# Encoder kernel on one core: small first inverse, TensorE kept at work before the projection, PSUM ring counted on at the end, tile 2's scores behind unit 0

## Chip, cores and metric

One Trainium2 chip, one core of it. The metric is the device time of one execution in microseconds (us). The kernel before takes 1320.02 us, the median of three runs.

## The reference

Pooled attention, then two feed-forward layers, all in float32. With q of 12288 rows by 128, kv of 384 x 32 positions by 128:

```
kv_pool = kv.reshape(B, 96, 4, 8, 4, C).mean(axis=(2, 4))     # 768 keys
k = v = kv_pool.reshape(B, 768, C) @ w_sr
a = softmax((q @ k.T) / sqrt(C))                              # sum + 1e-9
x = a @ v                                                     # 12288 x 128
h = x @ w_in1                                                 # 12288 x 2048
g = where(h >= 1, h, where(h <= -1, 0, (h + 1) ** 2 / 4))
y = g @ w_out1                                                # 12288 x 128
h2 = y @ w_in2
out = (h2 * sigmoid(1.702 * h2)) @ w_out2
```

## The kernel before

All tensors lie transposed: 128 channels or keys on the partitions, query rows along the free dimension. A query tile is T = 512 rows, there are NT = 24. Keys come in KC = 6 chunks of 128. The 2048 hidden features are taken as U = 8 units of 256, two blocks of 128 side by side in a 128x1024 PSUM buffer. A unit has a running number n = 8 * tile + unit.

A product that must be accurate is three TensorE passes of 512 columns (`three_passes`, L449 to L451): both operands are split in an upper part (float32r) and a lower remainder, and upper*upper, upper*lower and lower*upper are added up. The uppers are copies on ScalarE or VectorE; the lowers are subtractions, most of them on GpSimd (`lower`, L367: q_lo, k_lo, w_lo, g_lo, pt_lo). Early products (projections, values of tiles 0 to 2, layer 1's output for tile 0) are plain float32 instead, two instructions each.

**Order of the work.** There is no planner; each engine runs a program written out by hand, with semaphores between them. Iteration `it` holds, on TensorE, a block with the scores of tile `it` and the values of tile `it - 2`, and then eight steps k. A step has up to four parts: `layer_in` of layer 2 (h2), `layer_in` of layer 1 (h1, unit n = 8*it + k - 18), `layer_out` of layer 1 (two units behind) and `layer_out` of layer 2. ScalarE does Relu and Square of h1, and two passes of Gelu of h2; VectorE makes g1_hi and g1 (`unit_upper` L970, `unit_full` L979); GpSimd g1_lo and g2_lo. The last 11 units' g2_lo are VectorE's (TAIL). After the ramp, iterations 6 to 21 are a loop, and 22 to 27 are written out.

**PSUM.** Three buffers of 128x1024 form `ps_ring`; two of 128x512 (ps_y1, ps_y2) accumulate the layer outputs. h2 and h1 of step k take ring buffers `(2 + 2*k) % 3` and `(3 + 2*k) % 3`. The scores of a block use buffer 0, its values buffer 1. Since 16 is not a multiple of 3, the turn starts anew with each iteration: h1 of k = 7 and h2 of the next k = 0 both use buffer 2, with the block between them. In iterations 26 and 27 there is no block.

**Softmax.** Scores are copied to SBUF; VectorE takes the maximum over the keys in three `maximum` reductions and `fold_maximum`, which ends in max_turned; SP's queue writes it to DRAM and reads it back spread over all partitions (`spread_max`, key_max); VectorE's three `shift`s subtract it, ScalarE takes the exponentials, `add_keys` and `invert` make the inverse of the sums, which goes the same way through DRAM (`spread_inv`). `normalise` multiplies the values by it (x_sb), and x_hi and x_lo follow. Tile 0 goes another way: its maximum is spread by TensorE (`subtract_maximum` L503, with masked rows of `ident`), and its sums too, by one product with a matrix of ones, after which VectorE inverts all 128x512 of them (`normalise_first`).

**The ramp on each engine.** TensorE: key projection of the first 512 keys, value projection, scores of tile 0 (chunks 0 to 3), projections of the last 256 keys, chunks 4 and 5, scores of tile 1, `subtract_maximum`, values of tile 0 with the spread sums between chunks 3 and 4, steps of "iteration 2" (units 0 to 5), values of tile 1, scores of tiles 2 and 3, steps of iteration 3, and iteration 4. Layer 1's output of tile 1 (unit 8) can't start before y_lo of tile 0 has been taken out of ps_y1. VectorE sums the kv windows in 12 groups of 64 keys as they arrive, and then follows the order in the code at the end of its block. GpSimd: q_lo, k_lo, q_lo, w_lo of w_in1, then from x_lo of tile 0 on the other weights. ScalarE makes w_hi of w_in1 between the last value projection and the copies of tile 1's scores (`evacuate`).

## Time and profile before

| | |
|---|---|
| Median of three runs | 1320.02 us (1318.38 to 1321.22) |
| Profiled execution: time | 1320.54 us |
| Profiled execution: span | 1318.7 us |
| Mean granted TensorE clock | 0.994 |
| TensorE busy | 1274.6 us, 97% |
| GpSimd busy | 1145.5 us, 87% |
| ScalarE busy | 1007.7 us, 76% |
| VectorE busy | 1002.1 us, 76% |

PE is TensorE's matmuls, PEld its weight loads (which overlap them), DVE is VectorE, ACT ScalarE, POOL GpSimd, SPq the queue of SyncE. Times of the trace are us from the span's start. In a row of a time line, the first number is the start, the second how long the instruction or a run of like ones took, `xN` their count, and a bracket tells how long the engine was idle before, and which instruction ended the wait. Drawn matmul durations overlap; the distance between two starts is what a pass costs. A row of the table of stretches gives for each of PE, PEld, DVE, ACT and POOL the busy time and the instructions in brackets, then the granted TensorE clock, the DMA engines' share and GB/s.

### The profile page before, as it was taken

To read this page: it belongs to the slowest core of one execution; us is meant where nothing else is said; L and a number is where in the kernel's file an instruction comes from. 1 tells how busy PE (TensorE), PEld (TensorE's weight loads), DVE (VectorE), ACT (ScalarE), POOL (GpSimd) and SP (SyncE) were. 2 spreads that over 40 slices of the span, in tenths; PEclk is the share of its full clock that TensorE was granted. 3 is DMA by queue.
4 is the path that set the end of the run, shared out by engine and by line. 5 is a ranking of instruction groups with operands and counts; after the bars stand their busy time and mean duration, and the time that the engine had idled before them with its cause. 6 is when DMAs were issued, how large, how long until landed. Compare 5 with 4: busy or idle time off the path is not lost.

```text
span 1318.7 us, 16960 instructions
## 1 busy us (share of the span) xinstructions
PE 1274.6 (97%) x5468; PEld 1028.7 (78%) x5468; DVE 1002.1 (76%) x1146; ACT 1007.7 (76%) x1070; POOL 1145.5 (87%) x477
## 2 busy tenths in 40 slices
PE   4888999999999999999999999999999999999988
PEld 3446888888888888888888888888888888878866
DVE  6878779779788787797787887877978878756433
ACT  2567788887878887878778788878788787886756
POOL 2337999999999999999999999999999999998760
PEclk9998999999999999999999999999999999999999
DMA  9000000000010010000000000100000000000000
GB/s 347 22 17 24 17 17 32 16 17 17 16 32 16 16 32 16 16 31 17 16 16 16 32 16 16 32 16 16 28 20 16 16 17 25 9 17 17 1 8 17
DMA packets 18258, 35.72 MB, mean 27 GB/s; under 512 B 3248, under 2 KB 3376, under 8 KB 17968
## 3 DMA queue, kind: packets, MB, share of 16 engines
q1 hardware_dynamic: 18224, 35.30, 8.2%
q8 instruction: 18, 0.29, 0.1%
q14 instruction: 16, 0.13, 0.0%
HBM read 28.90 MB, written 6.39 MB: 27 GB/s over the span
## 4 chain that ended last, share of the span: by engine, by line
PE 82%; POOL 7%; issue 6%; DVE 3%; ACT 1%; DMA 1%; SPq 0%; POOLq 0%; ACTq 0%; DVEq 0%
PE ps_ring L449 16%; PE ps_ring L450 15%; PE ps_ring L451 15%; PE ps_y L449 11%; PE ps_y L451 11%; PE ps_y L450 11%; POOL g_lo L367 5%; POOL pt_lo L367 2%; DMA kv_sb<-in_kv_t 1%; PE ps_y L527 1%; PE ps_y L552 1%; DVE g L979 0%; DVE s_third L926 0%; DVE part_max L865 0%; DVE g_hi L970 0%
## 5 line engine op out<-in xcount | busy, mean ns | idle before, releaser
L367 POOL TENSOR_TENSOR g_lo<-g,g_hi 128x1024 fp32r<-128x1024 f32 x365 | 930.1, 2578 | 92.1 <-DVE g L979 86.7
L970 DVE SCALAR_TENSOR_TENSOR g_hi<-g,ps_ring 128x1024 fp32r<-128x1024 f32 x184 | 224.1, 1218 | 151.6 <-ACT g L768 150.7
L749 ACT ACTIVATE g<-ps_ring 128x1024 f32<-128x1024 f32 x192 | 197.2, 1027 | 182.8 <-PE ps_ring L451 178.6
L449 PE MATMUL ps_y<-g_hi,w_hi 128*128 128x512 f32 x752 | 297.0, 395 | 11.8 <-DVE y_lo L824 7.0
L450 PE MATMUL ps_y<-g_lo,w_hi 128*128 128x512 f32 x752 | 293.7, 391 | 0.0
L451 PE MATMUL ps_y<-g_hi,w_lo 128*128 128x512 f32 x752 | 293.7, 391 | 0.0
L979 DVE SCALAR_TENSOR_TENSOR g<-g,ps_ring 128x1024 f32<-128x1024 f32 x192 | 233.0, 1213 | 9.6 <-ACT g L768 9.6
L761 ACT ACTIVATE g<-ps_ring 128x1024 f32<-128x1024 f32 x192 | 197.9, 1031 | 17.0 <-PE ps_ring L451 10.4
L768 ACT ACTIVATE g<-g 128x1024 f32<-128x1024 f32 x192 | 204.2, 1063 | 5.4
L751 ACT ACTIVATE g_hi<-ps_ring 128x1024 fp32r<-128x1024 f32 x192 | 195.9, 1020 | 5.1 <-PE ps_y L451 5.1
L449 PEld LDWEIGHTS ps_y<-g_hi,w_hi 128*128 128x128 f32 x752 | 141.4, 188 | 49.7 <-POOL g_lo L367 10.6
L451 PEld LDWEIGHTS ps_y<-g_hi,w_lo 128*128 128x128 f32 x752 | 141.7, 188 | 29.9
L450 PEld LDWEIGHTS ps_y<-g_lo,w_hi 128*128 128x128 f32 x752 | 141.7, 188 | 28.3
L367 POOL TENSOR_TENSOR pt_lo<-s_sb,pt_hi 128x1024 fp32r<-128x1024 f32 x63 | 159.1, 2559 | 0.0
L449 PE MATMUL ps_ring<-x_hi,w_hi 128*128 128x512 f32 x384 | 153.5, 400 | 5.2 <-DVE x_lo L824 4.5
L449 PE MATMUL ps_ring<-y_hi,w_hi 128*128 128x512 f32 x384 | 150.9, 393 | 4.8 <-DVE g L979 4.8
L450 PE MATMUL ps_ring<-y_lo,w_hi 128*128 128x512 f32 x384 | 150.6, 392 | 0.0
L451 PE MATMUL ps_ring<-y_hi,w_lo 128*128 128x512 f32 x384 | 150.3, 391 | 0.0
L450 PE MATMUL ps_ring<-x_lo,w_hi 128*128 128x512 f32 x384 | 150.1, 391 | 0.0
L451 PE MATMUL ps_ring<-x_hi,w_lo 128*128 128x512 f32 x384 | 150.0, 391 | 0.0
L926 DVE TENSOR_TENSOR s_sb<-s_sb,key_max 128x1024 f32<-128x1024 f32 x66 | 124.5, 1889 | 0.0
L848 DVE COPY s_sb<-ps_ring 128x512 f32<-128x512 f32 x120 | 81.0, 689 | 54.6 <-PE ps_ring L451 54.6
(114 smaller groups left out, 1675.4 us busy)
## 6 DMA issues: line engine op xcount, KB each, us to landing
kv_sb<-in_kv_t SPq DMA_DIRECT2D x12, 512.0 KB, 8.6
q_sb<-in_q_t SPq DMA_DIRECT2D x24, 256.0 KB, 3.6
out_t<-y_sb SPq DMA_DIRECT2D x24, 256.0 KB, 3.6
key_max<-max_row SPq DMA_DIRECT2D x23, 256.0 KB, 3.4
inv_sum<-inv_row SPq DMA_DIRECT2D x23, 256.0 KB, 3.3
w_raw<-in_moe_w_in SPq DMA_DIRECT2D x2, 1024.0 KB, 17.7
max_row<-max_turned SPq DMA_DIRECT2D x23, 2.0 KB, 1.3
inv_row<-inv_turned SPq DMA_DIRECT2D x23, 2.0 KB, 1.3
```

The lines of the kernel that those rows point to most:

```text
L367: return nc.gpsimd.tensor_tensor(dst, src, upper.bitcast(F32), ALU.subtract)
L449: nc.tensor.matmul(dst, l_hi, r_hi, start=start, stop=False)
L450: nc.tensor.matmul(dst, l_hi, r_lo, start=False, stop=False)
L451: return nc.tensor.matmul(dst, l_lo, r_hi, start=False, stop=stop)
L749: nc.scalar.activation(g2[:, slot, :], ps_h2(k), ACT.Gelu_apprx_sigmoid).then_inc(g2_done, 1)
L751: nc.scalar.activation(g2_hi[:, slot, :], ps_h2(k), ACT.Gelu_apprx_sigmoid).then_inc(g2_hi_done, 1)
L761: nc.scalar.activation(g, ps_h1(k), ACT.Relu, bias=0.5, scale=0.5).then_inc(relu_done, 1)
L768: nc.scalar.activation(g, g, ACT.Square).then_inc(square_done, 1)
L848: nc.vector.tensor_copy(s_sb[:, half, c, :], ps_s(it, c)).then_inc(s_evac, 1)
L926: nc.vector.tensor_tensor(pair, pair, key_max[:, :].unsqueeze(1).to_broadcast([P, 2, T]), ALU.subtract).then_inc(shifted, 1)
L970: nc.vector.scalar_tensor_tensor(out=g1_hi[:, uu % 2, :], in0=g1[:, uu % 2, :], scalar=1.0, in1=ps_h1(k), op0=ALU.min, op1=ALU.max).then_i ...
L979: nc.vector.scalar_tensor_tensor(out=g, in0=g, scalar=1.0, in1=ps_h1(k), op0=ALU.min, op1=ALU.max).then_inc(g1_done, 1)
```

## The change

1. TensorE: ahead of the first key projection, behind each of window groups 4 to 7, two products of w_k with the first 256 window sums into an unused buffer. The result is not read.
2. Projection and scores of tile 0: k_lo of the first 512 keys in two halves; the projection of the last keys comes ahead of chunk 3; VectorE takes the maximum of chunk 0 alone, before k_lo of the last keys. w_hi of w_in1 is made by GpSimd, its first half before the maximum and its second after the maximum is masked. `ident` is 128x128.
3. First inverse: the key sums are added over the partitions by four products with one column each (128x4), inverted there, multiplied into the identity, and spread by one product with ones; ScalarE copies the result to inv_sum.
4. Unit 0 (`first_unit`) starts on x_hi, and adds the part with x_lo at the end. It needs only half of w_lo of w_in1.
5. Tile 2's scores stand behind unit 0, ahead of units 1 to 5, no longer behind tile 1's values. The maximum, shifts, key sums and exponentials of tile 2, and the order on SP, move forward to match.
6. Iterations 26 and 27 (`blockless`) count the ring on from iteration 25; h2 there waits for the unit before, not for the newest.
7. pt_lo of the last tile is made by VectorE (`last_probs_lower`), not GpSimd.

```diff
@@ names @@
+        def ring_turn(it, k):
+            return k + U * (it - NT - 1) if blockless(it) else k
+        def ps_h2(it, k):
+            return ps_ring[:, (2 + 2 * ring_turn(it, k)) % 3, :]
+        def ps_h1(it, k):
+            return ps_ring[:, (3 + 2 * ring_turn(it, k)) % 3, :]
+        def blockless(it):
+            return isinstance(it, int) and it >= NT + 2
@@ sync @@
+            spread_max(2)
             spread_inv(1)
-            spread_max(2)
@@ gpsimd @@
             def iteration(it, half):
-                if is_tile(it - 1):
+                if is_tile(it - 1) and not is_number(it, NT):
                     for p in range(PAIRS):
                         probs_lower(it - 1, 1 - half, p)
...
-            lower(k_lo[:, 0:FIRST_KEYS], k_sb[:, :], k_hi[:, 0:FIRST_KEYS]).then_inc(k_lo_first, 1)
+            for b in range(2):
+                keys = slice(b * FIRST_KEYS // 2, (b + 1) * FIRST_KEYS // 2)
+                lower(k_lo[:, keys], k_sb[:, keys], k_hi[:, keys]).then_inc(k_lo_first, 1)
             q_lower(1, q1_lo[:, :], q_sb[:, 1, :], q1_hi[:, :])
+            w_upper(0, 0)
             w_lower(0, 0)
+            pool.wait_ge(max_masked, 2)
+            w_upper(0, 1)
             w_lower(0, 1)
+            q_lower(2, q2_lo[:, :], q2_sb[:, :], q2_hi[:, :])
             pool.wait_ge(x_lo_done, 1)
@@ tensor @@
-                nc.tensor.matmul(ps_y2[:, :], ones[:, :], key_sums[:, 4, :], start=True,
+                for j in range(QUADS):
+                    last = nc.tensor.matmul(ps_y2[:, j:j + 1], key_sums[:, 4, j * P:(j + 1) * P], ones[:, 0:1],
+                                            start=True, stop=True)
+                last.then_inc(first_summed, 1)
+            def spread_inverse():
+                pe.wait_ge(inverse_masked, 1)
+                nc.tensor.matmul(ps_y2[:, :], ones[:, :], key_sums[:, 0, :], start=True,
                                  stop=True).then_inc(sums_spread, 1)
+            def first_unit(dst):
+                pe.wait_ge(w_lo_done[0], 1)
+                pe.wait_ge(x_hi_done, 1)
+                for d in range(2):
+                    f = slice(d * P, (d + 1) * P)
+                    half = dst[:, d * T:(d + 1) * T]
+                    nc.tensor.matmul(half, w_hi[:, f], x_hi[:, 0, :], start=True, stop=False)
+                    nc.tensor.matmul(half, w_lo[:, f], x_hi[:, 0, :], start=False, stop=False)
+                pe.wait_ge(x_lo_done, 1)
+                for d in range(2):
+                    f = slice(d * P, (d + 1) * P)
+                    last = nc.tensor.matmul(dst[:, d * T:(d + 1) * T], w_hi[:, f], x_lo[:, 0, :], start=False, stop=True)
+                last.then_inc(h1_ready, 1)
...
-                    if k == 0:
-                        at_least(pe, g1_done, it * U - 18 if unit(it, k - 1, FIRST1)[0] else NT * U)
+                    if blockless(it):
+                        pe.wait_ge(g1_done, min(it * U + k - 19, NT * U))
+                    elif k == 0:
+                        at_least(pe, g1_done, it * U - 18)
...
-                        at_least(pe, g1_done, it * U + k - 19 if layer1 else NT * U)
+                        at_least(pe, g1_done, it * U + k - 19)
...
             pe.wait_ge(w_scaled, 2)
+            for g in range(4, FIRST_GROUPS):
+                pe.wait_ge(summed, g)
+                for _ in range(2):
+                    nc.tensor.matmul(ps_k[:, 3, 0:4 * GK], w_k[:, :], window_sum[:, 0:4 * GK], start=True, stop=True)
             project_k(0)
             project_v(0)
-            for c in range(FIRST_CHUNKS):
+            for c in range(FIRST_CHUNKS - 1):
                 score_chunk(0, c)
             project_k(1)
+            score_chunk(0, FIRST_CHUNKS - 1)
             project_v(1)
...
-            spread_sums()
-            for c in range(4, KC):
-                value_chunk(0, c)
-            for k in range(U):
+            sum_first_keys()
+            value_chunk(0, 4)
+            spread_inverse()
+            value_chunk(0, 5)
+            for k in range(3):
                 step(2, 0, k)
-            values_then_scores(1, 2, 3)
+            for c in range(KC):
+                score_chunk(2, c)
+            pe.wait_ge(s_early, 2 * KC)
+            for k in range(3, U):
+                step(2, 0, k)
+            values_then_scores(1, 3)
@@ scalar @@
-            w_upper(0)
             evacuate(1, 1)
             for p in range(PAIRS):
                 exponential_first(p)
+            act.wait_ge(sums_spread, 1)
+            copy(inv_sum[:, :], ps_y2[:, :]).then_inc(inverse_copied, 1)
             copy(v_hi[:, :, :], v_sb[:, :, :]).then_inc(v_hi_done, 1)
             act.wait_ge(q2_loaded, 16)
             copy(q2_hi[:, :], q2_sb[:, :]).then_inc(q_hi_done, 1)
             step(2, 0, 2)
+            evacuate(2, 0)
@@ vector @@
+            def invert_first():
+                dve.wait_ge(first_summed, 1)
+                nc.vector.tensor_scalar(inv_first[:, :], ps_y2[:, 0:QUADS], 1e-9, None, ALU.add).then_inc(first_eps, 1)
+                dve.wait_ge(first_eps, 1)
+                nc.vector.reciprocal(inv_first[:, :], inv_first[:, :]).then_inc(first_inverse, 1)
...
-                nc.vector.tensor_scalar(inv_sum[:, :], ps_y2[:, :], 1e-9, None, ALU.add).then_inc(eps_added, 1)
-                nc.vector.reciprocal(inv_sum[:, :], inv_sum[:, :]).then_inc(inverted, 1)
...
+                if is_number(it, NT):
+                    for p in range(PAIRS):
+                        last_probs_lower(it - 1, 1 - half, p)
...
             unit_full(2, 2)
+            for p in range(PAIRS):
+                maximum(2, 0, p)
             unit_full(2, 3)
             shift(1, 1, 0)
             unit_full(2, 4)
             shift(1, 1, 1)
             shift(1, 1, 2)
             unit_full(2, 5)
+            fold_maximum(2)
...
             unit_full(2, 7)
-            for p in range(PAIRS):
-                maximum(2, 0, p)
-            fold_maximum(2)
             normalise(1)
             x_lower(1, 1)
+            for p in range(PAIRS):
+                shift(2, 0, p)
```

In iteration 3, VectorE's `shift`s of tile 2 fall away at k = 1 and 2, `fold_maximum(3)` moves from k = 2 to 1, the key sums of tile 2 from k = 4 to 2 and 3 (y_lo of tile 0 comes at the start of k = 3), and `invert(2)` from k = 5 to 4; ScalarE's three exponentials of tile 2 stand behind steps 0, 1 and 2 in place of all behind step 3.

## Rows read from the trace of the kernel before

**Rows 1.** The page, shares of the engines (busy us, share of the span, instructions)
```profile
PE 1274.6 (97%) x5468; PEld 1028.7 (78%) x5468; DVE 1002.1 (76%) x1146; ACT 1007.7 (76%) x1070; POOL 1145.5 (87%) x477
```

**Rows 2.** Table of stretches, 200 to 400 us
```profile
200.00:400.00 200.00, 200.00 (x881) 164.55 (x880) 161.02 (x187) 161.17 (x170) 192.29 (x79) 1.00 0.07 22
```

**Rows 3.** Time line of TensorE, ramp: start, us, instruction, idle before and its releaser
```profile
16.32 2.05 PE L456 MATMUL ps_k<-window_sum,w_k 128*128 128x512 f32 x2 [16.32 <-DVE window_sum L834]
...
20.97 0.77 PE L449 MATMUL ps_ring<-q_hi,k_hi 128*128 128x512 f32 x1 [0.90 <-POOL k_lo L367]
...
25.72 0.59 PE L456 MATMUL ps_k<-window_sum,w_k 128*128 128x256 f32 x2
26.15 0.61 PE L462 MATMUL ps_v<-w_v,window_sum 128*128 128x128 f32 x4
27.25 0.50 PE L449 MATMUL ps_ring<-q_hi,k_hi 128*128 128x512 f32 x1 [0.49 <-DVE k_lo L824]
...
33.93 1.62 PE L503 MATMUL ps_ring<-spread_hi,minus_ones 128*128 128x512 f32 x6 [0.33 <-DVE spread_hi L890]
...
48.22 0.50 PE L449 MATMUL ps_ring<-x_hi,w_hi 128*128 128x512 f32 x1 [4.50 <-DVE x_lo L824]
...
80.84 0.50 PE L449 MATMUL ps_ring<-x_hi,w_hi 128*128 128x512 f32 x1 [0.69 <-ACT s_sb L680]
...
101.95 0.80 PE L449 MATMUL ps_y<-g_hi,w_hi 128*128 128x512 f32 x1 [7.04 <-DVE y_lo L824]
...
115.10 0.47 PE L449 MATMUL ps_y<-g_hi,w_hi 128*128 128x512 f32 x1 [0.97 <-POOL g_lo L367]
```

**Rows 4.** Time line of ScalarE: score copies of tile 2
```profile
71.19 1.30 ACT L680 ACTIVATE s_third<-ps_ring 128x512 f32<-128x512 f32 x2 [3.67 <-PE ps_ring L451]
```

**Rows 5.** Time line of VectorE in the ramp
```profile
8.56 12.73 DVE L834 TENSOR_REDUCE window_sum<-kv_sb 128x64 f32<-128x1024 f32 x10 [0.89 <-DMA kv_sb<-in_kv_t]
...
31.52 1.47 DVE L885 CAST row_hi<-row_max 32x16 fp32r<-32x16 f32 x1
...
42.76 3.35 DVE L915 RECIPROCAL inv_sum<-inv_sum 128x512 f32<-128x512 f32 x1
...
62.80 3.49 DVE L932 TRANSPOSE_TENSOR_REDUCE part_sum<-s_sb 128x32 f32<-128x1024 f32 x3
...
69.78 0.24 DVE L950 RECIPROCAL row_sum<-row_sum 32x16 f32<-32x16 f32 x1
70.05 0.20 DVE L953 STREAM_TRANSPOSE inv_turned<-row_sum 32x32 f32<-32x32 f32 x1
...
90.99 1.21 DVE L926 TENSOR_TENSOR s_third<-s_third,key_max 128x1024 f32<-128x1024 f32 x1
...
95.51 4.50 DVE L926 TENSOR_TENSOR s_third<-s_third,key_max 128x1024 f32<-128x1024 f32 x2
```

**Rows 6.** Time line of GpSimd in the ramp
```profile
19.56 1.26 POOL L367 TENSOR_TENSOR k_lo<-k_sb,k_hi 128x512 fp32r<-128x512 f32 x1 [10.48 <-ACT k_sb L680]
...
104.23 2.38 POOL L367 TENSOR_TENSOR g_lo<-g,g_hi 128x1024 fp32r<-128x1024 f32 x1 [5.30 <-DVE g L979]
```

**Rows 7.** The page, DMA issues: count, KB each, us to landing
```profile
inv_sum<-inv_row SPq DMA_DIRECT2D x23, 256.0 KB, 3.3
...
inv_row<-inv_turned SPq DMA_DIRECT2D x23, 2.0 KB, 1.3
```

**Rows 8.** Time line of TensorE in the tail
```profile
1178.65 0.68 PE L449 MATMUL ps_y<-g_hi,w_hi 128*128 128x512 f32 x1 [2.02 <-POOL g_lo L367]
...
1264.51 0.80 PE L449 MATMUL ps_ring<-y_hi,w_hi 128*128 128x512 f32 x1 [2.35 <-DVE g L979]
...
1279.53 0.47 PE L449 MATMUL ps_ring<-y_hi,w_hi 128*128 128x512 f32 x1 [2.44 <-DVE g L979]
```

**Rows 9.** Time line of GpSimd in the tail
```profile
1168.69 7.59 POOL L367 TENSOR_TENSOR pt_lo<-s_sb,pt_hi 128x1024 fp32r<-128x1024 f32 x3
```

**Rows 10.** Time line of VectorE in the tail
```profile
1283.17 1.23 DVE L824 TENSOR_TENSOR g_lo<-g,g_hi 128x1024 fp32r<-128x1024 f32 x1 [3.78 <-ACT g_hi L751]
```

More of the change, by code:

```diff
@@ L963, in x_lower, with last_probs_lower @@
                 lower(x_lo[:, half, :], x_sb[:, :], x_hi[:, half, :]).then_inc(x_lo_done, 1)
+            def last_probs_lower(t, slot, p):
+                chunks = slice(2 * p, 2 * p + 2)
+                dve.wait_ge(pt_hi_done, (t - WHOLE) * PAIRS + (p + 1))
+                dve.wait_ge(pv_done, (t - 1) * KC + (2 * p + 2))
+                lower(pt_lo[:, chunks, :], s_sb[:, slot, chunks, :], pt_hi[:, chunks, :]).then_inc(pt_lo_last, 1)
             def unit_upper(it, k):
@@ L1054, in _ @@
             unit_full(2, 7)
-            for p in range(PAIRS):
-                maximum(2, 0, p)
-            fold_maximum(2)
             normalise(1)
             x_lower(1, 1)
+            for p in range(PAIRS):
+                shift(2, 0, p)
             for k in range(U):
```

130 lines of the change are left out of this document (73 added, 57 removed).

## The prediction

> **What bounds the kernel now.** I read the page first for the shares of the engines, then the table of stretches, then the time line of each engine through the first 145 us and the last 160 us. TensorE is busy for 97% of the span [rows 1]. In the table of stretches it is busy for all of 200 to 400 us, 881 instructions in 200 us, so one full 512-column pass in 0.227 us, at a granted clock of 1.00; GpSimd has 192.3 us of the 200 and follows close behind [rows 2]. The middle of the kernel is therefore TensorE's own work. The change leaves the loop's instructions as they are, so whatever it does to the time is made where TensorE stands or runs at the lower of its levels (1.2 instead of 2.4 GHz): the ramp to 115 us, and the tail from 1165 us. The time line of TensorE names these places. In the ramp: scores of tile 0 at about 0.4 us a pass between 20.97 and 25.72, the wait for x_lo before 48.22 (4.50 us), the run of twelve score chunks that ends with the wait before 80.84, the wait for y_lo before 101.95 (7.04 us) with a slow stretch behind it, and a wait for GpSimd before 115.10 [rows 3]. After 115.10 only about 1.5 us of waits are left up to the loop, so a gain at 115.10 stays. In the tail: three waits, before 1178.65, 1264.51 and 1279.53, the first two with passes at 0.43 us behind them [rows 8].
>
> **Part 1, up to the first maximum.** The change puts eight more weight-and-pass pairs (four groups, two products of 256 columns each) ahead of the first key projection. A 512-column projection at the low level takes 2.06 us less its drain, 1.7 us, from 16.32 [rows 3]; two of 256 columns cost the same, and the groups arrive from 11.1 us on, one per 1.27 us (ten reductions in 12.73 us from 8.56) [rows 5]. The slow stretches of before lasted 3.0 us (49.2 to 52.2) to 5.0 (101.95 to 106.9). Both ends: if this one is as short, the added products are done before 16.3; if it is as long, they end at 17.2 and push the projection back 0.9 us. I take 16.7. At the high level a projection of 512 columns is worth 1.05 us (256 columns: 0.63 us from 25.72 to ScalarE's copy) [rows 3], so k_hi starts at 17.75 in place of 18.40. The key halves on GpSimd cost 0.66 us each in place of 1.26 for all [rows 6], so score chunk 0 starts at 19.7 instead of 20.97. Three chunks of 0.69 us reach 21.8; the second key projection (its sums are there at 21.3) takes 0.43, chunk 3 0.69, the values' projection 0.5; ScalarE's copy and VectorE's k_lo end at 23.3 beside it. Chunk 4 starts at 23.4, before at 27.25: 3.85 us earlier. The six chunks of tile 1 are paced by ScalarE's copies (4.5 us in both) and end at 29.3. The chain of the maximum is ready by then: its last reduction ends at 26.3, and the cast of row_hi, which took 1.47 us beside GpSimd's w_lo [rows 5], meets only the end of the one w_lo half that is now ahead of it (27.65). The subtraction of the maximum thus starts at 29.3 instead of 33.93 [rows 3]: **4.65 us**.
>
> **Part 2, the first inverse.** The exponentials, value chunks and key sums move with it; the sums are ready at 36.1. Removed: 0.69 us of eps and 3.35 us of reciprocal on 128x512 [rows 5]. Added: eight loads with one column behind each. The nearest row is the projection of values with 128 columns, four instructions in 0.61 us [rows 3]: 0.12 to 0.19 us each by what of it is drain, so 0.9 to 1.5 us; I take 1.2, and 0.25 of drain. By the Trainium skill, "TensorE: Matmul & The Clock Gate", section LDWEIGHTS, a load is set by its columns over 1.2 GHz, which as an estimate makes 0.86 us of the eight; no row has such a product with one column. On VectorE 0.2 for eps and 0.2 for the reciprocal (32x16 took 0.24 [rows 5]), 0.7 for the masked 128x512 product; on TensorE another product of 1.15 us to landing, on ScalarE a 0.6 us copy. Value chunks 4 and 5 stand between them, and the last of those, at 41.0, ends last. x_hi starts at 41.0 in place of 46.15: **5.15 us** so far, so part 2 is worth 0.5 (0 to 1). Unit 0 no longer waits for x_lo: four passes at 41.75, two at 43.05 when x_lo is done (before, TensorE waited for it until 48.22), so unit 0 ends at 43.6.
>
> **Part 3, scores of tile 2 behind unit 0.** q_lo(2) is just in time: ScalarE copies the inverse (to 40.75), v_hi and q2_hi (42.1), GpSimd needs to 43.45. The first two chunks run at once, but ScalarE first does unit 0's Relu and Square (2.25 us); copies go in pairs of 1.3 us, chunk c+2 behind the copy of c [rows 4]. The last copy ends 6.95 us after 43.6, at 50.55, where unit 1 begins. TensorE gives away 2.8 us here. Units 1 to 5 and four layer-1 outputs follow as before; tile 1's values begin at 64.6 (before 65.3). Then only six chunks remain, not twelve: 5.4 us from 69.75 to the last copy, and unit 6 starts at 75.2 where it started at 80.84 [rows 3].
> Next late is VectorE. From 54.2 it has no gap: units 1 to 3 and three shifts to 61.3, the maximum of tile 2 (1.4 us) to 62.7, three key sums (3.49) [rows 5], unit 4, and the inverse of tile 1 (2.0 to 2.9), so inv_turned is ready at 69.3 to 70.2, hardly before the 70.25 of before [rows 5]. The inverse's two transfers take 4.7 us [rows 7], x_upper waits for ScalarE's last copy at 75.1, and x_lo is done at 76.4 to 77.1. Now the three shifts of tile 2 come first, at a time when GpSimd has nothing to do: 1.2 us each, against 4.50 for two beside GpSimd's g_lo [rows 5]. They end at 80.3; unit 6, two maxima, unit 7, maximum and fold of tile 3, unit 8 (2.3), two key sums end at 92.2, and y_lo at 92.9 (before 101.9). Unit 9 is through at 95.2, and GpSimd's g_lo of it, which waited for VectorE until 104.23 [rows 6], starts there; GpSimd then has no gap of note until TensorE's wait before 115.10: q_lo, g_lo, w_lo, g_lo of layer 2. It bounds this stretch, so TensorE reaches the 115.10 point at 106.3. Its stand from 89.1 to 93.3 may bring the low level back; up to some 2 us of that lie under GpSimd. **The ramp gives 8.8 us** (5.5 to 11).
>
> **Part 4, the tail.** Iteration 24: pt_lo of the last tile leaves GpSimd (7.59 us from 1168.69 [rows 9]) for VectorE, whose own such subtraction takes 1.23 us [rows 10]; it runs while GpSimd has no input (g2_hi comes at 1173.5) and delays x_lo by under 2 us, which nobody needs before 1178. GpSimd's g_lo is then done at 1175.95, before TensorE asks at 1176.5. The stand before 1178.65 with the slow passes to 1182.40 holds ten instructions in 6.16 us where 2.27 would do: 3.9 us. Two new short waits come behind: 0.2 for unit 174's result at 1177.9, 0.65 for GpSimd, which now takes g_lo of that unit first. **3.0 us** (2.2 to 3.9).
> Iteration 26: the waits before 1264.51 and 1279.53 are for VectorE's result of the unit just computed, in the ring slot that is written next [rows 8]. Counting on makes the slot that of the step before. With slow passes they cost 3.8 and 2.6 us. New: layer 1's last output needs GpSimd's g_lo of unit 191, which by its queue (2.4 us each) is about 0.8 us late. **5.6 us** (4.5 to 6.4).
>
> **Sum.** 8.8 + 3.0 + 5.6 = 17.4 us. The profiled execution has a span of 1318.7 and a time of 1320.54, 0.5 above the median of 1320.02; from the median, 1302.6 us.
>
> **Rivals.**
> A, the clock falls in the ramp. Between 41 and 51 us TensorE now works some 60% of the time, in pairs of chunks. For it: it was low at 49.2 after 4.5 us of standing and at 1179 after 2.0 us. Against: it stayed high across the 0.97 us before 115.10, and the largest new stand is 1.5 us. If it falls, 8 to 11 passes from 50.55 on cost 0.2 us more each, 2 us, and all behind them is that much later: 1304.6. The Trainium skill's "TensorE: Matmul & The Clock Gate", in the section on PSUM-queue depth-cycling, says that frequent short idles between groups of matmuls make the clock swing; that is this case, and speaks against the change. Chance 0.2.
> B, the tail's waits only move. If GpSimd or VectorE, next in line in each of the three places, is late by 1.5 us more than I laid out, the tail gives 4 us: 1307. For it: GpSimd is at 96% in the steady part; against: here it has one tile's pt_lo less. Chance 0.1.
> C, the ramp's gain is lost on VectorE: its queue from 54 to 95 us is full, and shifts slowed by GpSimd (1.5 us each instead of 1.2 to 3) or a late inverse keep y_lo after 97. Then the ramp gives 4: 1307.4. Chance 0.1.
> D, slower. TensorE stays at 1.2 GHz from unit 1 on, its work broken up by ScalarE's pace. Each pass there costs 0.2 us more; from 87 slow passes the whole 17.4 us are gone, and the some 140 instructions from 50.5 to 89 would make 28: 1331. Against: the longest slow stretch of before was 5.0 us. Chance 0.03.
> E, no part does anything (GpSimd, not TensorE, sets the pace, so an earlier start is spent in waiting): against it stand the 7.7 us that GpSimd is free in 200. 1320. Chance 0.03.
>
> **Numbers.** The forecast has 0.54. Its own range is 1299.5 to 1305; with A to C and the bounds of the parts (12 to 21 us in all) 1298 to 1308.5. A measurement of this kernel tells 0.2%, 2.6 us, from no change. Faster 0.94, within 0.03, slower 0.03.
>
> **What would show it.** Right: passes at 0.23 us in the first scores; the subtraction at about 29.3; x_hi at 41; unit 1 near 50.5; unit 6 near 75; shifts of tile 2 at 1.2 us; the first layer-1 output of tile 1 near 93 and no stand over 1 us in the three places of the tail. Wrong: slow passes after 44 us, VectorE's y_lo after 97, or a wait for GpSimd's g_lo at k = 2 of iteration 24 or k = 3 of iteration 26 that is over 2 us.

## The result, and the profile after

The changed kernel takes 1306.38 us (median of four runs, 1305.67 to 1306.85), the kernel before beside it 1319.41 (four runs, 1318.38 to 1321.22): a ratio of 0.9899, with a 95% interval of 0.9882 to 0.9916. It is faster by 13.0 us, where 17.4 were forecast; the time lies in the stated range of 1298.0 to 1308.5, above the forecast's own (1299.5 to 1305). The profiled execution has a span of 1305.0 in place of 1318.7, so 13.7 us are to be found in the trace.

The page's shares answer to [rows 1], the table of stretches, 200 to 400 us, to [rows 2].

```profile
PE 1273.4 (98%) x5492; PEld 1028.9 (79%) x5492; DVE 1003.5 (77%) x1151; ACT 1006.3 (77%) x1069; POOL 1139.7 (87%) x476
```

```profile
200.00:400.00 200.00, 200.00 (x881) 164.54 (x880) 160.85 (x184) 161.27 (x170) 191.18 (x77) 1.00 0.07 22
```

The middle is as before, 881 instructions in 200 us. The time line of TensorE in the ramp (start, us, instruction, idle before) answers to [rows 3].

```profile
17.48 1.02 PE L476 MATMUL ps_k<-window_sum,w_k 128*128 128x512 f32 x2
...
24.23 0.50 PE L469 MATMUL ps_ring<-q_hi,k_hi 128*128 128x512 f32 x1
...
30.41 1.52 PE L523 MATMUL ps_ring<-spread_hi,minus_ones 128*128 128x512 f32 x6
...
37.29 1.02 PE L532 MATMUL ps_y<-ones,key_sums 128*128 128x1 f32 x8
38.18 1.10 PE L554 MATMUL ps_y<-s_sb,v_sb 128*128 128x512 f32 x2
...
44.48 0.73 PE L589 MATMUL ps_ring<-x_lo,w_hi 128*128 128x512 f32 x2 [0.89 <-DVE x_lo L876]
...
48.41 0.50 PE L469 MATMUL ps_ring<-q_hi,k_hi 128*128 128x512 f32 x1 [1.82 <-ACT s_third L738]
...
52.43 0.51 PE L469 MATMUL ps_ring<-x_hi,w_hi 128*128 128x512 f32 x1 [0.69 <-ACT s_third L738]
...
95.38 0.80 PE L469 MATMUL ps_y<-g_hi,w_hi 128*128 128x512 f32 x1 [4.30 <-DVE y_lo L876]
...
108.49 0.77 PE L469 MATMUL ps_y<-g_hi,w_hi 128*128 128x512 f32 x1 [1.96 <-POOL g_lo L380]
...
111.61 0.53 PE L470 MATMUL ps_ring<-y_lo,w_hi 128*128 128x512 f32 x1
...
117.01 5.31 PE L554 MATMUL ps_ring<-s_third,v_sb 128*128 128x512 f32 x12
```

Read it against the rows of before by their distances. The subtraction of the maximum starts at 30.41 instead of 33.93, the first layer-1 output of tile 1 at 95.38 instead of 101.95 (its wait is 4.30 in place of 7.04), the layer-2 output behind it at 108.49 instead of 115.10. So TensorE is 6.6 us ahead there. The row at 117.01 starts the values of tile 2; the same values stood at 122.20 before, so there TensorE is 5.2 us ahead. The row at 108.49 ends a wait of 1.96 us, where before had 0.97 [rows 3]; behind it come eight passes a good 0.42 us apart, up to the row at 111.61, and then no wait up to 117.01. The loop then ends 5.1 us earlier on GpSimd (1143.66 for 1148.77). The rest of the 13.7, 8.6 us, is the tail's.

VectorE and ScalarE, time lines of the ramp; the first answers to [rows 5].

```profile
9.05 12.69 DVE L886 TENSOR_REDUCE window_sum<-kv_sb 128x64 f32<-128x1024 f32 x10 [1.10 <-DMA kv_sb<-in_kv_t]
...
38.35 0.16 DVE L977 TENSOR_SCALAR inv_first<-ps_y 128x4 f32<-128x4 f32 x1 [1.21 <-PE ps_y L532]
38.55 0.18 DVE L979 RECIPROCAL inv_first<-inv_first 128x4 f32<-128x4 f32 x1
...
41.60 0.69 DVE L989 TENSOR_TENSOR x_hi<-ps_y,inv_sum 128x512 fp32r<-128x512 f32 x1 [0.99 <-PE ps_y L554]
...
42.92 1.50 DVE L876 TENSOR_TENSOR x_lo<-x_sb,x_hi 128x512 fp32r<-128x512 f32 x1
...
79.61 3.49 DVE L997 TENSOR_TENSOR s_third<-s_third,key_max 128x1024 f32<-128x1024 f32 x3
...
94.68 0.64 DVE L876 TENSOR_TENSOR y_lo<-ps_y,y_hi 128x512 fp32r<-128x512 f32 x1
```

```profile
47.26 0.61 ACT L738 ACTIVATE q_hi<-q_sb 128x512 fp32r<-128x512 f32 x1
47.78 1.06 ACT L738 ACTIVATE s_third<-ps_ring 128x512 f32<-128x512 f32 x2
```

The row of ten reductions starts 0.49 us later than before (9.05 for 8.56): the reads of kv arrived later. In the 14 profiles of this study that start lies between 8.33 and 9.08, whatever the kernel. The early marks are best read from there.

GpSimd's time line in the ramp answers to [rows 6].

```profile
42.59 1.28 POOL L380 TENSOR_TENSOR q_lo<-q_sb,q_hi 128x512 fp32r<-128x512 f32 x1 [8.96 <-ACT q_hi L738]
...
97.66 2.39 POOL L380 TENSOR_TENSOR g_lo<-g,g_hi 128x1024 fp32r<-128x1024 f32 x1 [2.77 <-DVE g L1056]
100.01 1.30 POOL L380 TENSOR_TENSOR q_lo<-q_sb,q_hi 128x512 fp32r<-128x512 f32 x1
101.26 2.41 POOL L380 TENSOR_TENSOR g_lo<-g,g_hi 128x1024 fp32r<-128x1024 f32 x1
103.63 2.41 POOL L380 TENSOR_TENSOR w_lo<-w_raw,w_hi 128x1024 fp32r<-128x1024 f32 x1
105.99 14.75 POOL L380 TENSOR_TENSOR g_lo<-g,g_hi 128x1024 fp32r<-128x1024 f32 x5
```

From 97.66 to 120.7 it has no gap. Two of the five g_lo of the last row are slow ones:

```profile
108.31 3.37 POOL L380 TENSOR_TENSOR g_lo<-g,g_hi 128x1024 fp32r<-128x1024 f32 x1
111.64 3.46 POOL L380 TENSOR_TENSOR g_lo<-g,g_hi 128x1024 fp32r<-128x1024 f32 x1
```

The tail, on TensorE, VectorE and GpSimd, answers to [rows 8, 9]:

```profile
1177.70 0.50 PE L469 MATMUL ps_y<-g_hi,w_hi 128*128 128x512 f32 x1 [0.47 <-POOL g_lo L380]
...
1269.84 0.50 PE L469 MATMUL ps_y<-g_hi,w_hi 128*128 128x512 f32 x1 [0.73 <-POOL g_lo L380]
```

```profile
1162.77 4.20 DVE L876 TENSOR_TENSOR pt_lo<-s_sb,pt_hi 128x1024 fp32r<-128x1024 f32 x3 [0.35 <-ACT pt_hi L738]
```

```profile
1168.48 2.40 POOL L380 TENSOR_TENSOR g_lo<-g,g_hi 128x1024 fp32r<-128x1024 f32 x1 [4.87 <-ACT g_hi L803]
```

The three stands of about 2 us (a stand is a time in which TensorE waits) are gone with the slow passes behind them, and 0.47 and 0.73 us remain.

### The profile page after: what moved, and what is told of

The parts are those of the page before. It is cut to its first block, busy times and chain, and to the rows that moved or that the text cites. A ratio compares the mean times of both kernels' runs of the same rounds, so it can differ in the third digit from the quotient of the medians.

```text
span 1305.0 us, 17011 instructions
## 1 busy us (share of the span) xinstructions
PE 1273.4 (98%) x5492; PEld 1028.9 (79%) x5492; DVE 1003.5 (77%) x1151; ACT 1006.3 (77%) x1069; POOL 1139.7 (87%) x476
## 4 chain that ended last, share of the span: by engine, by line
PE 87%; POOL 5%; issue 4%; DVE 3%; ACT 1%; DMA 1%; POOLq 0%; SPq 0%; ACTq 0%; DVEq 0%
PE ps_ring L469 16%; PE ps_ring L471 16%; PE ps_ring L470 16%; PE ps_y L469 12%; PE ps_y L471 12%; PE ps_y L470 12%; POOL g_lo L380 4%; DVE g L1056 1%; DMA kv_sb<-in_kv_t 0%; PE ps_k L704 0%; DVE part_sum L1003 0%; POOL pt_lo L380 0%; PE ps_y L554 0%; DVE part_max L923 0%; DVE s_third L997 0%
## 5 line engine op out<-in xcount | busy, mean ns | idle before, releaser
L380 POOL TENSOR_TENSOR pt_lo<-s_sb,pt_hi 128x1024 fp32r<-128x1024 f32 x60 | 151.4, 2551 | 0.0
```

The lines of the kernel that those rows point to most:

```text
L380: return nc.gpsimd.tensor_tensor(dst, src, upper.bitcast(F32), ALU.subtract)
```

## The experiments

**Theory.** The tail gives what was forecast. The ramp gives less, for two causes: near 42 to 48 us GpSimd's q_lo of tile 2 and ScalarE's copies stand in each other's way and in x_lo's; and behind 97 us GpSimd's chain, not TensorE, sets the pace. **Rivals**: the low clock behind 108.49 is itself the loss; the move of tile 2's scores, or the added products, gives less than they should; the tail gave less than the trace says. The kernel before took 1318.11 us beside the first four kernels, 1318.72 beside the next four, 1319.39 beside the last four and 1319.41 beside the changed kernel. The changed kernel was not timed again beside the others, so a difference of a microsecond between it and one of them is not safe; kernels of the same group of four compare directly.

**The tail alone**, on the kernel before.

```diff
+        def ring_turn(it, k):
+            return k + U * (it - NT - 1) if blockless(it) else k
...
-                if is_tile(it - 1):
+                if is_tile(it - 1) and not is_number(it, NT):
...
+                if is_number(it, NT):
+                    for p in range(PAIRS):
+                        last_probs_lower(it - 1, 1 - half, p)
```

> The kernel before with the two tail parts alone: the ring counted on in iterations 26 and 27, and pt_lo of the last tile on VectorE. Ramp as before. My account of the two traces puts 5.1 us of the 13.7 us of span in the ramp and 8.6 in the tail (2.9 up to iteration 25, 5.7 behind it). If the tail parts act by themselves, this run is 8.6 us faster than before, about 1311, with its start and loop at the times of before. Rival: the tail's gain needs the GpSimd queue in the state in which the changed ramp leaves it; then it is 5 us or less.

It took 1311.32 us (1310.96 to 1313.80), a ratio of 0.9951 (0.9935 to 0.9968): 6.8 us, by the interval 4.2 to 8.6. The 8.6 expected is the interval's upper end.

```profile
1182.26 0.50 PE L456 MATMUL ps_y<-g_hi,w_hi 128*128 128x512 f32 x1 [0.45 <-POOL g_lo L374]
...
1274.40 0.50 PE L456 MATMUL ps_y<-g_hi,w_hi 128*128 128x512 f32 x1 [0.73 <-POOL g_lo L374]
```

The same two waits remain as in the changed kernel, 0.45 and 0.73 us. In this trace the tail gives 8.6 us of the 9.1 by which the span is shorter; the rest is an earlier ramp, although its instructions are those of before. What is left between this kernel and the changed one is the ramp: 4.9 us by the two times (1311.32 less 1306.38), 6.2 by the two gains (13.0 less 6.8), beside 5.1 in the trace.

**The ring alone**, without the edit of pt_lo.

```diff
+        def ring_turn(it, k):
+            return k + U * (it - NT - 1) if blockless(it) else k
...
+                    if blockless(it):
+                        pe.wait_ge(g1_done, min(it * U + k - 19, NT * U))
```

> The kernel before with the ring counted on in iterations 26 and 27 and nothing else. Expected: the two waits before 1264.51 and 1279.53 go, the one before 1178.65 stays with its slow passes; 5.7 us faster, about 1313.8. If instead the pt_lo move is what frees the tail (GpSimd late behind the ring), under 3 us.

1313.86 us (1312.05 to 1314.65), a ratio of 0.9964 (0.9952 to 0.9977), so 4.2 us, between 3.0 and 6.3. The wait in iteration 24 is still there:

```profile
1178.91 0.50 PE L455 MATMUL ps_y<-g_hi,w_hi 128*128 128x512 f32 x1 [2.01 <-POOL g_lo L373]
```

It is 2.01 us for GpSimd's g_lo, and the passes behind it stay 0.23 us apart, where before they ran slow [rows 8]. So the place costs 2.0 us in this profile, not the 3.9 of the profile of before: the clock's share of a stand varies. The two waits of iteration 26 are gone and give 5.7 us in the trace, as expected. The rest of the tail's gain hangs on pt_lo (2.5 us between this kernel and the tail alone). Both expected sizes lie in their intervals, 8.6 at the very edge, and by the times alone the tail could also have given 2 us less than the trace shows; its mechanism is shown, edit by edit.

**Tile 2's scores back** to where they stood, with their maximum, shifts and exponentials; all else as in the changed kernel.

```diff
-            for k in range(3):
-                step(2, 0, k)
-            for c in range(KC):
-                score_chunk(2, c)
-            pe.wait_ge(s_early, 2 * KC)
-            for k in range(3, U):
+            for k in range(U):
                 step(2, 0, k)
-            values_then_scores(1, 3)
+            values_then_scores(1, 2, 3)
...
```

> The changed kernel with the third tile's scores, copies, maximum, shifts, key sums and exponentials back at the places of the kernel before; everything else of the change stays. Theory A, the move pays by taking VectorE's shifts of tile 2 out of GpSimd's way and ahead of y_lo: y_lo comes 3 to 5 us later than in the changed kernel (98 to 100), and the run takes about 1310. Theory B, the move pays nothing: without it TensorE doesn't stand 5 us between units 0 and 1, unit 6 starts at 74.2 instead of 77.0, and with the 21.1 us from there to the first layer-1 output of before this comes at 95.3, as in the changed kernel; the run is within 1 us of 1306.4.

1306.62 us (1306.03 to 1307.10), a ratio of 0.9909 (0.9892 to 0.9925): its range overlaps the changed kernel's. The time lines of TensorE and GpSimd show where the move's advance ends.

```profile
96.82 0.80 PE L469 MATMUL ps_y<-g_hi,w_hi 128*128 128x512 f32 x1 [7.08 <-DVE y_lo L872]
```

```profile
112.12 2.40 POOL L380 TENSOR_TENSOR g_lo<-g,g_hi 128x1024 fp32r<-128x1024 f32 x1
```

The first layer-1 output of tile 1 is 1.4 us later than in the changed kernel (96.82 for 95.38), and so is the layer-2 output (109.96 for 108.49). But the wait there is 0.79, no slow pass follows, and the block's last scores stand at 126.42, against 126.22. GpSimd gives the reason. Its third g_lo of the chain, which the second layer-2 output needs, ends at 114.5 here and at 115.1 in the changed kernel, although the chain starts 1.4 us later (107.42 for 105.99). Here the second and third g_lo take 2.40 us each, in the changed kernel 3.37 and 3.46. There VectorE's shifts of tile 3, which the move has brought forward too, are already running when these two start (106.37 to 109.43 and 111.61 to 116.17). Here the first shift starts at 112.64, inside the third g_lo, and it is the shift that is slow (2.97 us). The move is real as far as 108 us, and its own side effect takes it back.

**Without the added products** ahead of the first key projection.

```diff
-            for g in range(4, FIRST_GROUPS):
-                pe.wait_ge(summed, g)
-                for _ in range(2):
-                    nc.tensor.matmul(ps_k[:, 3, 0:4 * GK], w_k[:, :], window_sum[:, 0:4 * GK], start=True, stop=True)
```

> The changed kernel without the eight products ahead of the first key projection. They ran at the low clock to the last and pushed the projection from about 16.8 to 17.48, so either they cost 0.7 us or what follows pays for it. If they pay: the projection starts at 16.8 but takes 2.0 us, the first score is at 20.3, its passes take 0.43 us and score chunk 4 starts at 26.4 instead of 24.23, and the run is 2.2 us slower, 1308.6. Rival: the clock rises in the first chunks anyway or the later chain has slack for it; then 1306 to 1307.

1307.00 us (1306.41 to 1309.09), a ratio of 0.9918 (0.9902 to 0.9935); its range overlaps the changed kernel's. The projection runs at the low level, and the first scores at the high one all the same:

```profile
16.34 2.05 PE L476 MATMUL ps_k<-window_sum,w_k 128*128 128x512 f32 x2 [16.34 <-DVE window_sum L882]
...
20.45 0.47 PE L469 MATMUL ps_ring<-q_hi,k_hi 128*128 128x512 f32 x1 [0.36 <-POOL k_lo L380]
...
108.45 0.47 PE L469 MATMUL ps_y<-g_hi,w_hi 128*128 128x512 f32 x1 [1.74 <-POOL g_lo L380]
...
115.07 0.50 PE L469 MATMUL ps_y<-g_hi,w_hi 128*128 128x512 f32 x1 [0.93 <-POOL g_lo L380]
```

Two things are to be seen. The first score took 0.77 in the profile of before [rows 3] and 0.47 here, behind the same projection at the same time; the tail-alone kernel, whose start is that of before, also shows 0.47 (its chunk 4 is at 25.71, not 27.25, with the reads 0.39 us later). So when the level rises isn't fixed by the program. The expectation's premise was wrong in one point: in the changed kernel the products didn't run low to the last. Their instructions start 0.43 us apart up to 16.04 and 0.21 apart from 16.41 on. And with no slow pass behind 108.45, a wait for GpSimd's g_lo of 0.93 us appears before 115.07, which the changed kernel doesn't have, and the values of tile 2 start at 116.57, 0.4 us before the changed kernel's: GpSimd is next in line behind the slow clock.

**Fill the gap before 108.49**: nine products on old data, not read, ahead of the first layer-2 output, so that TensorE doesn't stand there.

```diff
+                    if is_number(n, 0):
+                        for _ in range(9):
+                            nc.tensor.matmul(ps_y2[:, :], w_hi[:, 0:P], x_hi[:, 0, :], start=True, stop=True)
```

> The changed kernel with nine more products of tile 0's x_hi (2.04 us, result overwritten) in the gap before 108.49, where TensorE waits 1.96 us for GpSimd and then runs eight passes at the low clock. If the low clock is what eats the 1.4 us lost between 108.49 and the values of tile 2, these start at 115.6 and the run is 1.4 us faster, 1305.0. If GpSimd's chain of five g_lo (14.75 us from 105.99) is next in line, a wait appears before the second layer-2 output near 115.0 and only 0.4 to 0.5 us come back, as in the run without warm products, where the clock stayed high by itself.

1305.98 us (1305.55 to 1306.70), a ratio of 0.9903 (0.9886 to 0.9919). The eight slow passes, worth 8 x 0.2 = 1.6 us by themselves, are gone from there, and only 0.4 us comes back at the block's last scores (125.84 for 126.22), and 0.4 in the time. By itself this run proves little: behind 95.26 there are 14 slow passes here, not 6, so the nine products ran late, from 107.76 to 109.80, and held the layer-2 output up 1.3 us longer than the wait had; the expected wait near 115 didn't appear. What rules out the rival that the low clock is the loss is the run before: there TensorE stood 1.74 us, no pass behind was slow, and the wait for g_lo (0.93) took the place of the slow passes but for 0.4 us.

**ScalarE's order**: the copies for v_hi and q2_hi ahead of the wait for the spread inverse, so that GpSimd's q_lo(2) is done before x_lo; and the copy for tile 3's q_hi behind those of tile 2's scores.

```diff
-            act.wait_ge(sums_spread, 1)
-            copy(inv_sum[:, :], ps_y2[:, :]).then_inc(inverse_copied, 1)
             copy(v_hi[:, :, :], v_sb[:, :, :]).then_inc(v_hi_done, 1)
             act.wait_ge(q2_loaded, 16)
             copy(q2_hi[:, :], q2_sb[:, :]).then_inc(q_hi_done, 1)
+            act.wait_ge(sums_spread, 1)
+            copy(inv_sum[:, :], ps_y2[:, :]).then_inc(inverse_copied, 1)
             step(2, 0, 2)
             evacuate(2, 0)
+            q_upper(3, 1)
...
-                if k == 2 and is_tile(it + 1):
+                if k == 2 and is_tile(it + 1) and not is_number(it, 2):
```

> The changed kernel with ScalarE's copies v_hi and q2_hi in its 5.4 us of waiting for the spread inverse, not behind it, and the copy q_hi of tile 3 behind the copies of tile 2's scores, not ahead. Theory: two waits that I had not laid out cost the ramp 1.3 us: x_lo of tile 0 took 1.50 us in place of 0.69 because GpSimd's q_lo(2) had started beside it, and the q_hi copy held the score copies by 0.5. Expected x_lo 0.7 us long, unit 1 at 51.1 instead of 52.4, y_lo 1.3 us earlier, the run 1 to 1.3 us faster if VectorE carries it on to GpSimd's g_lo chain; 0 to 0.3 if GpSimd's chain after 108.5 absorbs it.

1304.78 us (1304.69 to 1305.47), a ratio of 0.9895 (0.9878 to 0.9911): 1.6 us less than the changed kernel, 0.9 by the gains over the kernel before beside each. VectorE's and TensorE's time lines:

```profile
41.58 0.69 DVE L990 TENSOR_TENSOR x_hi<-ps_y,inv_sum 128x512 fp32r<-128x512 f32 x1 [0.99 <-PE ps_y L554]
...
42.90 0.69 DVE L877 TENSOR_TENSOR x_lo<-x_sb,x_hi 128x512 fp32r<-128x512 f32 x1
```

```profile
51.07 0.50 PE L469 MATMUL ps_ring<-x_hi,w_hi 128*128 128x512 f32 x1 [0.69 <-ACT s_third L738]
```

From x_hi to unit 1 it is 9.5 us (41.58 to 51.07), as the prediction had it (41.0 to 50.55); in the changed kernel it is 10.8 (41.60 to 52.43).

**GpSimd's order**: the last w_lo half of layer 1's output weights before the first g_lo, in a time when GpSimd stands, not between the g_lo.

```diff
             for k in range(U):
-                step(3, k)
-                if k == 4:
+                if k == 2:
                     pool.wait_ge(g1_used, PLAIN)
                     w_lower(1, 1)
+                step(3, k)
```

> The changed kernel with GpSimd's last w_lo of layer 1's output weights (2.4 us) ahead of the first g_lo, in its 15 us of idleness, not in its chain of g_lo. Theory: between 97.7 and 120.7 us GpSimd bounds. Then the first layer-2 output comes at 106.4 instead of 108.49, TensorE hardly waits and its clock stays high, the values of tile 2 start 2.4 to 3.7 us earlier, and the run is 2 to 3.5 us faster, 1303 to 1304.5. Rival: VectorE with its two slowed shifts (3.06 and 4.56 us) is as late as GpSimd and bounds the start of iteration 4; then under 1 us.

1304.19 us (1304.00 to 1304.23), a ratio of 0.9890 (0.9874 to 0.9907): 2.2 us less than the changed kernel, 1.5 by the gains. TensorE and GpSimd:

```profile
95.36 0.80 PE L469 MATMUL ps_y<-g_hi,w_hi 128*128 128x512 f32 x1 [4.26 <-DVE y_lo L876]
...
112.26 0.50 PE L469 MATMUL ps_y<-g_hi,w_hi 128*128 128x512 f32 x1 [0.29 <-POOL g_lo L380]
113.76 5.31 PE L554 MATMUL ps_ring<-s_third,v_sb 128*128 128x512 f32 x12
```

```profile
89.79 2.40 POOL L380 TENSOR_TENSOR w_lo<-w_raw,w_hi 128x1024 fp32r<-128x1024 f32 x1 [12.82 <-PE ps_y L595]
```

All is as in the changed kernel up to 95.36. Then 2.40 us less of GpSimd's work stand ahead of the layer-2 output, the wait of 1.96 and its slow passes are gone, and the values of tile 2 start at 113.76 instead of 117.01. From 97 us to these values GpSimd sets the pace, all but the 0.4 us of the clock.

**Both orders together**: the two diffs above, in one kernel.

```diff
+            q_upper(3, 1)
...
-                if k == 4:
+                if k == 2:
```

> Both edits: ScalarE's order and the early w_lo. If each acts on its own link of one chain (VectorE up to y_lo, GpSimd behind it), their gains add up: 3.3 to 4.8 us faster than the changed kernel, about 1302. If one bounds only when the other does, no more than the larger of the two.

1302.04 us (1301.57 to 1302.68), a ratio of 0.9876 (0.9859 to 0.9892), the fastest kernel here: 4.3 us less than the changed one (3.7 by the gains). The three kernels were timed beside each other, and there ScalarE's order is worth 2.2 us (1304.19 less 1302.04) and GpSimd's 2.7 (1304.78 less 1302.04). TensorE's time line:

```profile
50.45 0.50 PE L469 MATMUL ps_ring<-x_hi,w_hi 128*128 128x512 f32 x1 [0.69 <-ACT s_third L738]
...
75.06 0.50 PE L469 MATMUL ps_ring<-x_hi,w_hi 128*128 128x512 f32 x1 [0.69 <-ACT s_sb L738]
...
93.34 0.50 PE L469 MATMUL ps_y<-g_hi,w_hi 128*128 128x512 f32 x1 [4.22 <-DVE y_lo L877]
...
111.78 5.31 PE L554 MATMUL ps_ring<-s_third,v_sb 128*128 128x512 f32 x12
```

These are the forecast's marks (unit 1 at 50.55, unit 6 at 75.2, the first layer-1 output of tile 1 near 93): with ScalarE's order mended, the model of the ramp holds up to there. Behind, it doesn't: the first layer-2 output comes at 104.73, not at 106.3, and the values of tile 2 are 10.4 us ahead of before where the forecast had 8.8, because the w_lo that was moved was part of the forecast's chain. That the time is within 0.6 us of the 1302.6 forecast is therefore in part luck.

**Four kernels on GpSimd's new order.** First that kernel again, as their base, unchanged.

> The changed kernel with GpSimd's last w_lo half ahead of its first g_lo, again, as the base for the three kernels beside it. 1304.2 us as before.

1304.14 us (1303.36 to 1304.87); the first time it had 1304.19. So the one kernel that was timed on two occasions repeats to 0.05 us, while the kernel before moved by 0.7 between them; that speaks for the differences of the times over those of the gains.

The scores of tile 2 back at their old place, on that base:

```diff
-            for c in range(KC):
-                score_chunk(2, c)
...
-            values_then_scores(1, 3)
+            values_then_scores(1, 2, 3)
```

> The base with the scores of tile 2, their maximum, shifts and exponentials at the places of the kernel before. With the changed kernel's own queue on GpSimd the move of the scores was worth nothing: the layer-2 output at 108.49 came 1.45 us earlier with it, and the marks behind 126 were equal. Theory A, GpSimd's five g_lo swallowed that: with the last w_lo half out of their way the 1.4 us of the move come through, and this kernel takes 1.0 to 1.5 us more than the base, 1305.5. Theory B, the move is worth nothing whatever GpSimd does, since VectorE has the same work before y_lo either way: 1304.2, and the first layer-2 output within 0.3 us of the base's.

1304.84 us (1304.42 to 1305.90), 0.7 more, with ranges that overlap. The first layer-1 output of tile 1 comes 1.4 us later than the base's (96.04 for 94.67), and the values of tile 2 0.2 later (114.15 for 113.94), where the base had fourteen slow passes from 94.67 on. This lies between the two theories. The times don't decide, and the move is worth at most some 1 us.

The first inverse as before, on that base:

```diff
-                for j in range(QUADS):
-                    last = nc.tensor.matmul(ps_y2[:, j:j + 1], key_sums[:, 4, j * P:(j + 1) * P], ones[:, 0:1],
-                                            start=True, stop=True)
-                last.then_inc(first_summed, 1)
+                nc.tensor.matmul(ps_y2[:, :], ones[:, :], key_sums[:, 4, :], start=True,
+                                 stop=True).then_inc(first_summed, 1)
...
+                nc.vector.tensor_scalar(inv_sum[:, :], ps_y2[:, :], 1e-9, None, ALU.add).then_inc(first_eps, 1)
+                dve.wait_ge(first_eps, 1)
+                nc.vector.reciprocal(inv_sum[:, :], inv_sum[:, :]).then_inc(inverse_copied, 1)
```

> The base with the first inverse as in the kernel before (one product of the key sums with ones, eps and the reciprocal over 128x512, no copy on ScalarE). Theory A, the small inverse is worth what x_hi shows, some 1.0 us, in the ramp: x_hi at 42.6 and the time 1305.2. Theory B, a start of unit 0 that is 1 us later is lost behind it, because ScalarE's copies of tile 2's scores pace unit 1 and have one copy less ahead of them here: 1304.2.

1304.96 us (1303.97 to 1305.58), 0.8 more than the base, again with ranges that overlap. VectorE and TensorE of it:

```profile
38.48 3.35 DVE L974 RECIPROCAL inv_sum<-inv_sum 128x512 f32<-128x512 f32 x1
41.86 0.69 DVE L979 TENSOR_TENSOR x_hi<-ps_y,inv_sum 128x512 fp32r<-128x512 f32 x1
```

```profile
42.70 0.77 PE L582 MATMUL ps_ring<-x_hi,w_hi 128*128 128x512 f32 x1 [3.27 <-DVE x_hi L979]
43.27 0.63 PE L583 MATMUL ps_ring<-x_hi,w_lo 128*128 128x512 f32 x1
...
52.85 0.50 PE L469 MATMUL ps_ring<-x_hi,w_hi 128*128 128x512 f32 x1 [0.69 <-ACT s_third L735]
```

x_hi is 1.0 us later than in the base (41.86 for 40.85; counted from each one's first score, 0.9), and unit 1 1.2 later (52.85 for 51.68; 1.1). So an edit here does reach unit 1. It is worth 0.9 us at x_hi, where the prediction had 0.5.

**Both orders, without the added products.**

```diff
-            for g in range(4, FIRST_GROUPS):
-                pe.wait_ge(summed, g)
-                for _ in range(2):
-                    nc.tensor.matmul(ps_k[:, 3, 0:4 * GK], w_k[:, :], window_sum[:, 0:4 * GK], start=True, stop=True)
```

> Both re-orderings (ScalarE's copies, GpSimd's last w_lo half), without the eight added products ahead of the first key projection. Theory A, those products bring the high level 1 us earlier and this shows now that nothing behind them waits on GpSimd: 1303 to 1303.5. Theory B, the level rises by itself before the first scores, and the projection at the low level starts earlier by what it takes longer: 1302.0, with the first score within 0.2 us of that of the kernel with them.

1302.60 us (1302.29 to 1303.14), a ratio of 0.9873 (0.9856 to 0.9889); the kernel with the products had 1302.04, on another occasion, where before took 1318.72 and not 1319.39. Its reads came 0.49 us later (9.06 for 8.57). Counted from there, x_hi stands at 32.9 without and at 32.4 with the products. They are worth some 0.5 us at x_hi in these two profiles, and no time tells them from nothing. But in both profiles of the changed start without them the level rose before the first scores; in the profile of before it rose only at 25 us. What the products save in such an execution no run here shows.

## Why the prediction was right or wrong

**The tail: right.** 8.6 us were forecast (3.0 and 5.6). The trace shows 2.9 in iteration 24 and 5.7 in iteration 26, and the wait left for GpSimd's g_lo of unit 191 is 0.73 us, forecast 0.8. The tail alone, timed, gave 6.8 (4.2 to 8.6). Two details: pt_lo took 4.20 us for three on VectorE where 1.23 each were counted, and harmed nobody; and the two new short waits, forecast at 0.85 us together, cost 0.9 by the distances of the starts (0.1 and 0.8).

**Up to x_hi: right in the sum.** x_hi at 41.60 for 41.0; counted from the arrival of kv, the gain is 5.04 us where 5.15 were forecast. Its parts were off against each other. Part 1 gave 4.0 (counted so), not 4.65: the added products ended at 17.5 and not at 16.7, beyond the upper end of 17.2, just under it counted from the reads. And part of the 4.0 is luck of the profile of before: in the tail-alone kernel, which has the old start, the first scores ran high by themselves, and the subtraction of the maximum stood 1.9 us earlier than before, counted from the reads (32.39 less 8.95 for 33.93 less 8.56). The forecast put that difference down to the added products; without them it was there too (e4_no_warm, 30.31 less 8.55, only 0.4 later than in the changed kernel). Part 2 gave 1.0, not 0.5: eight one-column products took 0.9 us, from 37.29 to 38.18, where 1.2 were taken. The Trainium skill ("TensorE: Matmul & The Clock Gate", LDWEIGHTS) gives 0.85 us for these eight loads, as an estimate (eight times 128 columns over 1.2 GHz; the prediction has 0.86); the trace agrees.

**Unit 0 to unit 1: 1.3 us missed.** "x_lo is done" at 43.05 and "the last copy ends 6.95 us after 43.6" failed. x_lo took 1.50 us and not 0.69, because GpSimd's q_lo(2) ran from 42.59 to 43.87, and VectorE got through only behind it. The prediction had worked out that q_lo(2) would end at 43.45, and did not ask what it would run beside. The Trainium skill ("SBUF — State Buffer", Who interferes with whom) says that a VectorE instruction with two SBUF inputs contends with a GpSimd instruction that reads SBUF, and one with a single SBUF input does not; the trace agrees: x_lo has two; x_sb just ahead of it, with one operand in PSUM, ran beside the first 0.3 us of q_lo(2) and took its usual 0.68. The other half is ScalarE's copy for tile 3's q_hi, 0.61 us at 47.26, which stood in the queue ahead of the first copy of the scores and was left out of the count. The new order on ScalarE gives both back: 9.5 us from x_hi to unit 1, and 1.6 to 2.2 us in the time. It changes both places at once, so each half is read from the trace and not timed alone.

**"A gain at 115.10 stays": the step that failed.** TensorE reached that point 6.6 us earlier (8.8 forecast, less 1.3, the 0.5 of the reads and about 0.5 more on VectorE), and kept 5.2. The prediction said that GpSimd bounds the stretch, and then counted only up to its first product. Behind q_lo, g_lo and w_lo stand five more g_lo, 14.75 us without a gap from 105.99. Whether TensorE stands and runs slow (1.96 us and eight passes), or stays at the high level and stands again before 115 (0.93 us), the end is nearly the same: the block's last scores at 126.22 in the changed kernel, at 125.78 without the added products. Of the 1.4 us, 0.4 is the clock and 1.0 is GpSimd's: from the start of the five g_lo to the end of the third it takes 9.1 us (105.99 to 115.10), in the kernel before 8.1 (112.55 to 120.66), because two of the three were slowed beside VectorE's shifts of tile 3 and not one. This is read from the traces; no run moves those shifts alone. The prediction asked what the shifts of tile 2 would run beside, and left out those of tile 3, which move with them. Taking 2.40 us out of that chain moved the values of tile 2 by 3.25 us: the third g_lo ends 2.9 us earlier (112.2), for it is no longer slowed, and the 0.4 us of the clock is gone as well.

**So the ramp** gave 5.1 us: of the 8.8, 1.3 were lost between 42 and 52 us, 1.4 behind 108.49, and 0.5 is the late arrival of this profile's reads, no part of the change. The last 0.5 arises on VectorE between unit 1 (1.9 late) and y_lo (done at 95.3 for 92.9). There the inverse of tile 1 took 3.4 us (69.78 to 73.19) where 2.0 to 2.9 were allowed, and x_lo of tile 1, which waits for it, was done at 79.7 and not at 76.4 to 77.1; that this is the cause is not shown.

**Rivals.** A: no slow pass between 44 and 52 us in the changed kernel, though TensorE stood 0.89, 1.82 and 0.69 us there. The rule that it named from the Trainium skill ("TensorE: Matmul & The Clock Gate", the section on PSUM-queue depth-cycling), that frequent short idles make the clock swing, is thus not borne out by these stands. The mechanism is there all the same when the stand is longer: with the old inverse, behind 3.27 us, the passes from 43.27 to 47.5 are 0.43 apart. B: no. C, in the place it named: y_lo at 94.68, not after 97, and the three shifts of tile 2 took 3.49 us as forecast; but its size, a ramp worth 4, was near the truth, because another engine's queue did what VectorE's was suspected of. The move of tile 2's scores gave nothing measurable. D: no. E: not for the whole kernel, but its mechanism, an earlier start that is spent in waiting for GpSimd, is what took the 1.0 us behind 108.49.

## What to carry to other kernels

When a gain at one point is said to stay, follow the engine that ends last there until it next has a gap, not only to the first thing that it releases: here five instructions behind that point decided. When work is moved, write down for every instruction that moves with it what it will now run beside and whose queue it stands in; the two orders that mend two such places cost no work and give some 4 us. And read early marks from the arrival of the first data, since that alone moved by 0.75 us between profiles.

## What the runs showed of the hardware

The moment at which TensorE's granted clock rises is not a function of the program alone: kernels with the same start ran the first scores at the low level (before, the ring alone) or at the high one (the tail alone). With the eight added products the rise came among or at the end of them: in the changed kernel their instructions lie 0.43 us apart up to 16.04 and 0.21 apart from 16.41 on, and with the scores back on GpSimd's new order 0.21 apart already from 14.29, so that the key projection began at 16.27 and not at 17.48. Nor does a stand of a given length decide: 1.96 us before 108.49 was followed by eight slow passes, 1.74 before 108.45 and 2.01 before 1178.91 by none; and behind the stand of 4.3 us before tile 1's first layer-1 output, the kernel with GpSimd's new order, profiled twice, ran 6 slow passes once and 14 the other time. What decides between them stays open.

VectorE and GpSimd slow each other in both directions when VectorE subtracts two SBUF operands. A 128x1024 g_lo on GpSimd takes 2.40 us, and 3.37 and 3.46 where a shift of VectorE was running at its start; a shift takes 1.21 us, and 2.97 where it starts inside a g_lo.
